# First MLP: on VectorE h times n of a tile follows the last Mish operation of the preceding tile; ScalarE copies x2 out behind the Exp of a group's last tile

## The chip, the cores and the metric

One core of a Trainium2 chip runs the whole program. The metric is the time of one execution on the device in microseconds (us), the median of the runs. TensorE (PE in the profile) multiplies, VectorE (DVE), ScalarE (ACT) and GpSimd (POOL) do the elementwise work, and SyncE (SP) issues most of the transfers.

## The reference, cut to what matters

```
x  = attention(q, k, v)            # 1536 tokens x 512, causal band of local keys and global keys
h  = x @ w_in                      # 512 -> 2048
g  = h * tanh(log1p(exp(h)))       # Mish
x2 = g @ w_out                     # 2048 -> 512
p  = domain_probs / sum(domain_probs)
for e in 4 experts:                # 512 -> 1024 -> 512
    out += p[:, e] * (relu(x2 @ w1[e]) @ w2[e])
```

The change lies in the first MLP alone, the three lines from h to x2.

## The kernel before

Each float32 matrix product is made from float16 high and low parts, as three products (high by high, high by low, low by high). After the attention, `rest` runs on every engine. The 1536 tokens form 3 groups (NG) of 512, and the 2048 columns of h form 16 tiles (FT) of 128; a tile of the first MLP is one of these 16 column tiles for one group, [128 x 512], so there are 48 (STEPS). All engines run the same loop, `for T in range(STEPS + LAG)` with LAG = 6, and each is in step T at a time of its own. Nothing is scheduled by a tool: every engine's order is the order of the code, and semaphores tie the engines together.

What is done for tile T, and in which step of which engine:

- PE, step T: the first product, 12 matmuls of 512 columns (L608), into PSUM bank T % 4. It waits until L1353 of tile T-4 has read that bank (b_ready).
- ACT, step T: L973, u = exp(h). DVE, step T: L1347, u = min(u, U_MAX); L1349, n = (u + 2) u; L1353, g = -h n, which reads h from PSUM and n from SBUF.
- ACT, step T+1: L989, r = ln(n + 2), and L991, r = exp(-r). DVE, step T+1: L1365 and L1367, one Newton step on r.
- POOL, in its own loop: L816, g = g r, as soon as L1367 of the tile is done. Its result is g of the tile.
- ACT, step T+2: L983, the float16 high part of g. DVE, step T+2: L1359, its low part.
- PE, step T+6: the second product, 12 matmuls (L677), which adds the tile's share of x2 into four PSUM banks of their own. It waits for L1359 (h_ready).

With the last tile of a group (tiles 15, 31, 47, at step 21, 37, 53) the four banks hold x2 of the group. `take_x2` has ACT copy them to SBUF (L946, four copies). The second product of the next group's first tile (tile 16 at step 22, tile 32 at step 38) waits for each bank's copy before it writes the bank (x2_taken).

Between these, DVE has extra work at the end of certain steps: in steps 6, 8, ... 20 one reduction over a piece of the first expert's weights (L1070), in step 8 also the four small operations of `shares`, in steps 22 to 25 and 38 to 41 the largest value of x2 (L1298), in step 25 and 29 some small scale computations, in steps 31 to 34 the low parts of x2 (L1290), in steps 33, 35, 40 and 42 low parts of expert weights (L1323). At steps 1 and 3 it makes low parts of x for groups 1 and 2 (L1216); the second product of tile 0 waits for the last of these.

After the loop the experts follow, nearly all of it matmuls (L608).

Of the kernel before, what the change touches and what calls it, by code (L numbers as in the profile page):

```python
# [17 lines left out]
ALU = mybir.AluOpType  # L18
# [18 lines left out]
def program(nc, q, k, v, n_global, n_local, w_in, w_out, probs, w1, w2, out):  # L37
# [7 lines left out]
    FT = FF // P  # L45
# [3 lines left out]
    NG = N // GN  # L49
# [23 lines left out]
    with ExitStack() as ctx:  # L73
# [30 lines left out]
        def psum(i, n=GN, at=0):  # L104

            c = 512 * (i % 2) + at
            return bank[i // 2][:, c:c + n]
# [87 lines left out]
        u_t, n_t, r_t, g_t = temps[0:2], temps[2:4], temps[4:6], temps[6:10]  # L195
# [76 lines left out]
        u_ready, n_step, n_ready, b_ready = sem("u_ready"), sem("n_step"), sem("n_ready"), sem("b_ready")  # L272
# [3 lines left out]
        g_ready, h_hi, h_ready = sem("g_ready"), sem("h_hi"), sem("h_ready")  # L276
# [16 lines left out]
        STEPS = NG * FT  # L293
        LAG = 6
# [10 lines left out]
        W0_LOW = [T + 1 for T in W0_HIGH[:PIECES // 2]] + W0_HIGH[PIECES // 2:]  # L305


        TAKE_X2 = [FT + LAG - 1]
        TAKE_X2_LATE = {2 * FT + LAG - 1: 1}
        X2_SCALE = 7  # L310
        X2_HIGH = 8

# [519 lines left out]
        def _(act):  # L832
# [98 lines left out]
            def rest(banded):  # L931
# [8 lines left out]
                def take_x2(g):  # L940

                    for c in range(DC):
                        act.wait_ge(x2_psum, DC * g + c + 1)
                        if g and c == 0:
                            act.wait_ge(x_ready, XN + DC * g)
                        act.copy(y32[:, c], psum(4 + c)).then_inc(x2_taken, 1)  # L946
# [17 lines left out]
                act.wait_ge(inv_ready, 1)  # L964

                for T in range(STEPS + LAG):
                    if T in TAKE_X2:
                        take_x2(TAKE_X2.index(T))
                    if T < STEPS:
                        act.wait_ge(h_psum, T + 1)  # L970
                        if T >= 2:
                            act.wait_ge(n_ready, T - 1)
                        act.activation(u_t[T % 2], psum(T % 4), ACT.Exp, scale=inv_h).then_inc(u_ready, 1)  # L973
                    else:
                        expert_high(0, 0, T - STEPS)
                    if T in TAKE_X2_LATE:
                        take_x2(TAKE_X2_LATE[T])
                    if 0 <= T - 2 < STEPS:
                        m = T - 2
                        act.wait_ge(g_ready, m + 1)  # L980
                        if m >= RING:
                            act.wait_ge(l2_done, m - RING + 1)
                        act.activation(hv[:, m % RING, 0, :], g_t[m % 4], ACT.Copy).then_inc(h_hi, 1)  # L983
                    if 0 <= T - 1 < STEPS:
                        m = T - 1
                        act.wait_ge(n_ready, m + 1)
                        if m >= 2:
                            act.wait_ge(g_ready, m - 1)
                        act.activation(r_t[m % 2], n_t[m % 2], ACT.Ln, bias=two).then_inc(l_ready, 1)  # L989
                        act.wait_ge(l_ready, m + 1)  # L990
                        act.activation(r_t[m % 2], r_t[m % 2], ACT.Exp, scale=-1.0).then_inc(r_ready, 1)  # L991
                    if T in TURN_AT:
                        for c in range(DC):
                            x_high(TURN_AT[T], c)
                    ready = x2_due(T, X2_HIGH)
                    if ready and ready[1] < DC:
                        x2_high(*ready)
                    if T in W0_HIGH:
                        expert_0_high(W0_HIGH.index(T))
# [18 lines left out]
        def _(dve):  # L1018
# [256 lines left out]
            def rest():  # L1275
# [67 lines left out]
                for T in range(STEPS + LAG):  # L1343
                    if T < STEPS:
                        u, n = u_t[T % 2], n_t[T % 2]
                        dve.wait_ge(u_ready, T + 1)
                        dve.tensor_scalar(u, u, U_MAX, None, ALU.min).then_inc(n_step, 1)  # L1347
                        dve.wait_ge(n_step, T + 1)
                        dve.scalar_tensor_tensor(n, u, 2.0, u, ALU.add, ALU.mult).then_inc(n_ready, 1)  # L1349
                        if T >= 4:  # L1350
                            dve.wait_ge(h_ready, T - 3)
                        dve.wait_ge(n_ready, T + 1)
                        dve.scalar_tensor_tensor(g_t[T % 4], psum(T % 4), -1.0, n, ALU.mult, ALU.mult).then_inc(b_ready, 1)  # L1353
                    else:
                        expert_low(0, 0, T - STEPS)
                    if 0 <= T - 2 < STEPS:
# [4 lines left out]
                    if 0 <= T - 1 < STEPS:  # L1361
                        m = T - 1
                        n, r = n_t[m % 2], r_t[m % 2]
                        dve.wait_ge(r_ready, m + 1)
                        dve.scalar_tensor_tensor(e_t, n, 2.0, r, ALU.add, ALU.mult).then_inc(e_ready, 1)  # L1365
                        dve.wait_ge(e_ready, m + 1)
                        dve.scalar_tensor_tensor(r, e_t, 2.0, r, ALU.subtract, ALU.mult).then_inc(q_ready, 1)  # L1367
                    if T in TURN_AT:
                        for c in range(DC):
                            x_low(TURN_AT[T], c)  # L1370
# [95 lines left out]
```

## Time and profile before

| | us |
|---|---|
| median of 3 runs (lowest to highest) | 910.69 (910.62 to 911.55) |
| the profiled execution, its own time | 911.57 |
| its span (first to last instruction) | 909.7 |
| PE busy | 874.2 (96%) |
| DVE busy | 501.0 (55%) |
| ACT busy | 316.3 (35%) |
| POOL busy | 263.6 (29%) |

The shares are averages over stages of different kinds: attention up to about 150 us, the first MLP from there to about 424 us, the experts to the end. Times in the rows below are microseconds from the start of the span. In a timeline a row is one instruction or several alike: start, duration, engine, line and operation, out<-in, count, and in brackets how long the engine stood idle before it and who released it. Durations on DVE and ACT overlap a little: the next instruction can start before the one in front has ended, so steps are best measured from start to start.

### The profile page before, as it was taken

To read this page: it belongs to the slowest core of one execution; us is meant where nothing else is said; L and a number is where in the kernel's file an instruction comes from. 1 tells how busy PE (TensorE), PEld (TensorE's weight loads), DVE (VectorE), ACT (ScalarE), POOL (GpSimd) and SP (SyncE) were. 2 spreads that over 40 slices of the span, in tenths; PEclk is the share of its full clock that TensorE was granted. 3 is DMA by queue.
4 is the path that set the end of the run, shared out by engine and by line. 5 is a ranking of instruction groups with operands and counts; after the bars stand their busy time and mean duration, and the time that the engine had idled before them with its cause. 6 is when DMAs were issued, how large, how long until landed. Compare 5 with 4: busy or idle time off the path is not lost.

```text
span 909.7 us, 12637 instructions
## 1 busy us (share of the span) xinstructions
PE 874.2 (96%) x4916; PEld 443.7 (49%) x4916; DVE 501.0 (55%) x1010; ACT 316.3 (35%) x597; POOL 263.6 (29%) x218
## 2 busy tenths in 40 slices
PE   6878999899999999999999999999999999999998
PEld 6666776444444444444444444444444444444443
DVE  7665887999999999984641224322134322212121
ACT  4798886544554555463020111101020101101020
POOL 1368993222222232220009400068000193000000
PEclk9898999999999999999999999999999999999999
DMA  9771320000000000202000400000400000000001
GB/s 222 244 251 39 124 99 1 1 1 1 1 7 3 1 1 1 93 3 93 4 6 0 180 6 1 6 0 8 177 1 2 4 0 0 1 24 23 35 12 49
DMA packets 52004, 39.19 MB, mean 43 GB/s; under 512 B 40816, under 2 KB 41712, under 8 KB 51440
## 3 DMA queue, kind: packets, MB, share of 16 engines
q1 hardware_dynamic: 49888, 34.31, 12.6%
q10 hardware_dynamic: 2064, 4.19, 1.3%
q8 instruction: 31, 0.51, 0.2%
q14 instruction: 21, 0.17, 0.1%
HBM read 35.35 MB, written 3.15 MB: 42 GB/s over the span
## 4 chain that ended last, share of the span: by engine, by line
PE 70%; DVE 20%; ACT 7%; issue 2%; POOL 0%; DVEq 0%; ACTq 0%
PE bank L608 58%; PE bank L677 5%; DVE tmp L1349 4%; DVE tmp L1367 3%; DVE xT L1365 3%; PE bank L547 2%; DVE tmp L1347 2%; PE bank L579 2%; ACT scaled L866 2%; DVE tmp L1353 2%; PE bank L598 2%; DVE hid L1359 1%; ACT tmp L989 1%; ACT tmp L850 1%; ACT tmp L891 1%
## 5 line engine op out<-in xcount | busy, mean ns | idle before, releaser
L962 ACT ACTIVATE hid<-bank 128x512 f16<-128x512 f32 x96 | 57.2, 596 | 413.8 <-PE bank L608 413.8
L608 PE MATMUL bank<-xT,wA 128*128 128x512 f16 (+1 forms) x864 | 194.6, 379 | 0.0
L1340 DVE SCALAR_TENSOR_TENSOR hid<-bank,hid 128x512 f16<-128x512 f32 x96 | 66.3, 691 | 177.2 <-ACT hid L962 177.2
L677 PE MATMUL bank<-hid,wB 128*128 128x512 f16 x576 | 133.8, 383 | 5.4 <-ACT acc L946 4.2
L608 PEld LDWEIGHTS bank<-xT,wA 128*128 128x128 f16 x864 | 84.5, 98 | 100.7 <-issue 0.2
L608 PE MATMUL bank<-wA,hid 128*128 128x512 f16 x576 | 125.3, 379 | 0.0
L608 PE MATMUL bank<-wB,hid 128*128 128x512 f16 x576 | 125.3, 379 | 0.0
L608 PE MATMUL bank<-xT,wB 128*128 x576 | 125.3, 379 | 0.0
L816 POOL TENSOR_TENSOR tmp<-tmp 128x512 f32<-128x512 f32 x48 | 67.8, 1412 | 195.8 <-DVE tmp L1367 195.8
L771 POOL TENSOR_SCALAR stage<-stage,sc 128x1024 f32<-128x1024 f32 x32 | 35.8, 1120 | 255.1 <-DVEq L1333 245.3
L1418 DVE SCALAR_TENSOR_TENSOR acc<-bank,pg,acc 128x512 f32<-128x512 f32 x36 | 27.0, 751 | 131.7 <-PE bank L608 131.7
L677 PEld LDWEIGHTS bank<-hid,wB 128*128 128x128 f16 x576 | 56.6, 99 | 75.2 <-DVE hid L1359 5.2
L608 PEld LDWEIGHTS bank<-wB,hid 128*128 128x128 f16 x576 | 56.4, 98 | 68.0
L608 PEld LDWEIGHTS bank<-xT,wB 128*128 128x128 f16 x576 | 56.4, 98 | 68.0
L608 PEld LDWEIGHTS bank<-wA,hid 128*128 128x128 f16 x576 | 56.3, 98 | 68.0
L983 ACT ACTIVATE hid<-tmp 128x512 f16<-128x512 f32 x48 | 30.3, 630 | 116.5 <-POOL tmp L816 116.5
L1231 DVE SCALAR_TENSOR_TENSOR tmp<-bank,tmp 128x384 f16<-128x384 f32 (+2 forms) x96 | 47.0, 490 | 34.2 <-ACT tmp L891 33.1
L608 PE MATMUL bank<-xT,hid 128*128 (+1 forms) x288 | 63.6, 379 | 0.0
L579 PE MATMUL bank<-ident,tmp 128*128 128x128 f32 x240 | 45.7, 290 | 8.7 <-DVE tmp L1231 6.6
L850 ACT ACTIVATE tmp<-tmp 128x288 f32<-128x288 f32 (+2 forms) x96 | 48.6, 507 | 15.5 <-DVE tmp L1120 14.4
L1349 DVE SCALAR_TENSOR_TENSOR tmp<-tmp 128x512 f32<-128x512 f32 x48 | 52.1, 1086 | 1.6
L608 PEld LDWEIGHTS bank<-xT,hid 128*128 128x128 f16 x288 | 28.2, 98 | 34.0
(111 smaller groups left out, 940.8 us busy)
## 6 DMA issues: line engine op xcount, KB each, us to landing
stage<-in_moe_w SPq DMA_DIRECT2D x8, 2048.0 KB, 9.9
stage<-in_moe_w_in SPq DMA_DIRECT2D x1, 4096.0 KB, 14.5
wB<-in_moe_w_out ACTq DMA_DIRECT2D x1, 4096.0 KB, 15.9
hid<-in_q SPq DMA_DIRECT2D x16, 192.0 KB, 3.3
hid<-in_k SPq DMA_DIRECT2D x16, 192.0 KB, 3.4
xT<-in_v SPq DMA_DIRECT2D x8, 384.0 KB, 4.9
out_y<-acc SPq DMA_DIRECT2D x12, 256.0 KB, 2.0
rows<-max SPq DMA_DIRECT2D x4, 128.0 KB, 3.8
```

The lines of the kernel that those rows point to most:

```text
L579: last = pe.transpose(dst[:, b * P:(b + 1) * P], src[:, b * P:(b + 1) * P], ident[:])
L608: last = pe.matmul(dst, lhs(c, a), rhs(c, b), start=(c == 0 and n == 0), stop=(c == chunks - 1 and n == 2))
L677: last = pe.matmul(psum(4 + d), w_out_s[:, a, f // 2, f % 2, d * P:(d + 1) * P], hv[:, T % RING, b, :], start=(f == 0 and n == 0), stop=(f ...
L771: pool.tensor_scalar(tmp, src, scale, 1.0, ALU.mult, ALU.mult).then_inc(w_part, 1)
L816: pool.tensor_tensor(g_t[T % 4], g_t[T % 4], r_t[T % 2], ALU.mult).then_inc(g_ready, 1)
L850: act.activation(t, t, ACT.Exp, bias=nmax[:, u:u + 1], scale=-1.0).then_inc(p_ready, 1)
L962: act.activation(hv[:, f, 0, :], psum(f % 4), ACT.Relu).then_inc(f_hi, 1)
L983: act.activation(hv[:, m % RING, 0, :], g_t[m % 4], ACT.Copy).then_inc(h_hi, 1)
L1231: dve.scalar_tensor_tensor(pt[:, 1], src, P_SCALE, pt[:, 0], ALU.mult, ALU.subtract).then_inc(pT_dve, 1)
L1340: dve.scalar_tensor_tensor(hv[:, f, 1, :], psum(f % 4), 0.0, hv[:, f, 0, :], ALU.max, ALU.subtract).then_inc(f_ready, 1)
L1349: dve.scalar_tensor_tensor(n, u, 2.0, u, ALU.add, ALU.mult).then_inc(n_ready, 1)
L1365: dve.scalar_tensor_tensor(e_t, n, 2.0, r, ALU.add, ALU.mult).then_inc(e_ready, 1)
```

## The change

On VectorE, L1353 (h times n of tile T) with its two waits moves inside step T from its place behind L1349 to a place behind L1359 and the two Newton operations L1365 and L1367 of tile T-1, and ahead of all of the step's extra work. On ScalarE, the four copies of x2 of group 0 move behind the Exp L973 of step 21; those of group 1 already stand behind the Exp of step 37, and stay there.

```diff
-        TAKE_X2 = [FT + LAG - 1]
-        TAKE_X2_LATE = {2 * FT + LAG - 1: 1}
+        TAKE_X2_AT = [(g + 1) * FT + LAG - 1 for g in range(NG - 1)]
...
                 for T in range(STEPS + LAG):
-                    if T in TAKE_X2:
-                        take_x2(TAKE_X2.index(T))
                     if T < STEPS:
                         act.wait_ge(h_psum, T + 1)
...
                         expert_high(0, 0, T - STEPS)
-                    if T in TAKE_X2_LATE:
-                        take_x2(TAKE_X2_LATE[T])
+                    if T in TAKE_X2_AT:
+                        take_x2(TAKE_X2_AT.index(T))
...
                         dve.scalar_tensor_tensor(n, u, 2.0, u, ALU.add, ALU.mult).then_inc(n_ready, 1)
-                        if T >= 4:
-                            dve.wait_ge(h_ready, T - 3)
-                        dve.wait_ge(n_ready, T + 1)
-                        dve.scalar_tensor_tensor(g_t[T % 4], psum(T % 4), -1.0, n, ALU.mult, ALU.mult).then_inc(b_ready, 1)
...
                         dve.scalar_tensor_tensor(r, e_t, 2.0, r, ALU.subtract, ALU.mult).then_inc(q_ready, 1)
+                    if T < STEPS:
+                        if T >= 4:
+                            dve.wait_ge(h_ready, T - 3)
+                        dve.wait_ge(n_ready, T + 1)
+                        dve.scalar_tensor_tensor(g_t[T % 4], psum(T % 4), -1.0, n_t[T % 2], ALU.mult, ALU.mult
+                                                 ).then_inc(b_ready, 1)
                     if T in TURN_AT:
```

The order on VectorE of two steps of the first MLP, one that ends with a weight reduction and the next, in the kernel before (L1353 is h times n):

```order
L1367 SCALAR_TENSOR_TENSOR tmp<-xT,tmp 128x512
L1070 TENSOR_REDUCE wpieces<-stage 128x1
L1347 TENSOR_SCALAR tmp<-tmp 128x512
L1349 SCALAR_TENSOR_TENSOR tmp<-tmp 128x512
L1353 SCALAR_TENSOR_TENSOR tmp<-bank,tmp 128x512
L1359 TENSOR_TENSOR hid<-tmp,hid 128x512
L1365 SCALAR_TENSOR_TENSOR xT<-tmp 128x512
L1367 SCALAR_TENSOR_TENSOR tmp<-xT,tmp 128x512
L1347 TENSOR_SCALAR tmp<-tmp 128x512
L1349 SCALAR_TENSOR_TENSOR tmp<-tmp 128x512
```

And the same place in the changed kernel, where the lines of before have new numbers: L1347 is L1344, L1349 is L1346, L1359 is L1352, L1365 is L1358, L1367 is L1360, L1070 is L1067, and h times n, L1353 before, is L1365 now:

```order
L1360 SCALAR_TENSOR_TENSOR tmp<-xT,tmp 128x512
L1365 SCALAR_TENSOR_TENSOR tmp<-bank,tmp 128x512
L1067 TENSOR_REDUCE wpieces<-stage 128x1
L1344 TENSOR_SCALAR tmp<-tmp 128x512
L1346 SCALAR_TENSOR_TENSOR tmp<-tmp 128x512
L1352 TENSOR_TENSOR hid<-tmp,hid 128x512
L1358 SCALAR_TENSOR_TENSOR xT<-tmp 128x512
L1360 SCALAR_TENSOR_TENSOR tmp<-xT,tmp 128x512
L1365 SCALAR_TENSOR_TENSOR tmp<-bank,tmp 128x512
L1344 TENSOR_SCALAR tmp<-tmp 128x512
```

The one operation that reads a PSUM bank has moved from between n and the low part of g to directly behind the last Newton operation, ahead of the reduction where there is one.

The order on ScalarE at step 21, where x2 of group 0 is copied out (L946), before:

```order
L991 ACTIVATE tmp<-tmp 128x512
L946 COPY acc<-bank 128x512 x4
L973 ACTIVATE tmp<-bank,sc 128x512
L983 ACTIVATE hid<-tmp 128x512
L989 ACTIVATE tmp<-tmp,sc 128x512
```

And now, with L988 for L991, L970 for L973, L945 for L946, L980 for L983 and L986 for L989:

```order
L988 ACTIVATE tmp<-tmp 128x512
L970 ACTIVATE tmp<-bank,sc 128x512
L945 COPY acc<-bank 128x512 x4
L980 ACTIVATE hid<-tmp 128x512
L986 ACTIVATE tmp<-tmp,sc 128x512
```

The Exp and the four copies have changed places; at step 37 the order is the latter in both kernels.

## Rows read from the trace of the kernel before

**Rows 1.** Windows: busy time (and instructions) of each engine, TensorE clock, DMA share, GB/s
```profile
339.00:347.00 8.00, 4.66 (x14) 1.83 (x15) 7.66 (x11) 6.83 (x12) 1.58 (x2) 0.79 0.00 0
424.00:909.00 485.00, 482.21 (x2235) 218.39 (x2232) 141.72 (x224) 57.20 (x96) 102.52 (x72) 1.00 0.08 25
```

**Rows 2.** Timeline of PE at the copies of group 0
```profile
252.29 2.75 PE L608 MATMUL bank<-xT,wA 128*128 128x512 f16 x12
255.93 2.75 PE L677 MATMUL bank<-hid,wB 128*128 128x512 f16 x12 [0.88 <-ACT acc L946]
258.51 2.75 PE L608 MATMUL bank<-xT,wA 128*128 128x512 f16 x12
```

**Rows 3.** Timeline of PE at the copies of group 1
```profile
336.21 2.75 PE L608 MATMUL bank<-xT,wA 128*128 128x512 f16 x12
...
342.34 4.44 PE L677 MATMUL bank<-hid,wB 128*128 128x512 f16 x12 [3.37 <-ACT acc L946]
...
346.61 2.75 PE L608 MATMUL bank<-xT,wA 128*128 128x512 f16 x12
```

**Rows 4.** Timeline of ACT at the copies of groups 0 and 1
```profile
255.22 2.03 ACT L946 COPY acc<-bank 128x512 f32<-128x512 f32 x4
257.11 0.72 ACT L973 ACTIVATE tmp<-bank,sc 128x512 f32<-128x512 f32 x1
...
341.62 2.04 ACT L946 COPY acc<-bank 128x512 f32<-128x512 f32 x4
```

**Rows 5.** Timeline of DVE and POOL, a step that ends with a reduction
```profile
246.14 0.69 DVE L1367 SCALAR_TENSOR_TENSOR tmp<-xT,tmp 128x512 f32<-128x512 f32 x1
246.75 1.21 DVE L1070 TENSOR_REDUCE wpieces<-stage 128x1 f32<-128x1024 f32 x1
...
246.91 1.27 POOL L816 TENSOR_TENSOR tmp<-tmp 128x512 f32<-128x512 f32 x1 [3.47 <-DVE tmp L1367]
...
247.88 0.58 DVE L1347 TENSOR_SCALAR tmp<-tmp 128x512 f32<-128x512 f32 x1
...
248.50 0.69 DVE L1349 SCALAR_TENSOR_TENSOR tmp<-tmp 128x512 f32<-128x512 f32 x1
...
250.50 0.68 DVE L1365 SCALAR_TENSOR_TENSOR xT<-tmp 128x512 f32<-128x512 f32 x1
```

**Rows 6.** Timeline of DVE, POOL and ACT, the plain step behind it
```profile
251.22 0.69 DVE L1367 SCALAR_TENSOR_TENSOR tmp<-xT,tmp 128x512 f32<-128x512 f32 x1
251.83 0.42 DVE L1347 TENSOR_SCALAR tmp<-tmp 128x512 f32<-128x512 f32 x1
251.99 1.38 POOL L816 TENSOR_TENSOR tmp<-tmp 128x512 f32<-128x512 f32 x1 [3.81 <-DVE tmp L1367]
...
252.28 1.64 DVE L1349 SCALAR_TENSOR_TENSOR tmp<-tmp 128x512 f32<-128x512 f32 x1
...
253.40 0.63 ACT L983 ACTIVATE hid<-tmp 128x512 f16<-128x512 f32 x1 [2.71 <-POOL tmp L816]
...
254.03 0.69 DVE L1353 SCALAR_TENSOR_TENSOR tmp<-bank,tmp 128x512 f32<-128x512 f32 x1
254.63 0.68 DVE L1359 TENSOR_TENSOR hid<-tmp,hid 128x512 f16<-128x512 f32 x1
254.68 0.63 ACT L991 ACTIVATE tmp<-tmp 128x512 f32<-128x512 f32 x1
...
255.34 0.69 DVE L1365 SCALAR_TENSOR_TENSOR xT<-tmp 128x512 f32<-128x512 f32 x1
```

**Rows 7.** Timeline of DVE and POOL at step 1, low parts of x
```profile
158.51 2.48 DVE L1216 TENSOR_TENSOR xT<-bank,xT 128x512 f16<-128x512 f32 x4
158.67 1.27 POOL L816 TENSOR_TENSOR tmp<-tmp 128x512 f32<-128x512 f32 x1 [15.34 <-DVE tmp L1367]
```

**Rows 8.** Waits from 145 to 450 us
```profile
PE bank L677 <- DVE xT L1216: 1.2, 1, 1.2
```

**Rows 9.** Timeline of DVE at step 31, behind a low part of x2 (L1290)
```profile
314.25 1.49 DVE L1347 TENSOR_SCALAR tmp<-tmp 128x512 f32<-128x512 f32 x1
```

## The prediction, made before the changed kernel was run

> **What bounds the kernel now.** I read the windows first. From 424 us to the end PE is busy for 482.21 of 485.00 us at full clock [rows 1], and nothing that the change touches lies there: that part moves as a block with the end of the first MLP. So only idle PE time before 424 us can be won. The timeline of PE shows how much there is. From one first product to the next, with a second product between, PE takes (336.21 - 258.51) / 15 = 5.18 us per step [rows 2, 3], and that is its own pace, with no gap inside. Two steps are longer. Around the second product of tile 16: 258.51 - 252.29 = 6.22 us, so **1.04 us** is lost, behind a wait for the x2 copies L946 [rows 2]. Around that of tile 32: 346.61 - 336.21 = 10.40 us, so **5.22 us** is lost [rows 3]. Of this, 3.37 us is again the wait for L946; then the 12 matmuls take 4.27 us instead of 2.59, since the granted clock, 1.00 elsewhere, has a mean of 0.79 in this window [rows 1]: after the idle time it is at the lower of its two levels (1.2 against 2.4 GHz) for a while. Both waits are for ACT, and ACT is late because DVE, POOL and ACT together run behind PE. How late is seen in the copies: the first group's start at 255.22 us and the second's at 341.62 [rows 4], while PE wants the first bank at 252.29 + 2.59 = 254.88 and at 336.21 + 2.59 = 338.80 us. The start of the MLP holds 1.2 us more, a wait of the first second product for L1216 [rows 8]. So the pace of the DVE-POOL-ACT group up to step 37 decides, and PE's own pace after that.
>
> **What paces DVE, POOL and ACT.** A step that ends with a reduction takes 251.22 - 246.14 = 5.08 us from L1367 to L1367 [rows 5, 6]. The plain one behind it takes 255.34 - 251.22 = 4.12 us up to L1365, and L1367 follows L1365 by 0.72 us [rows 5, 6], so 4.84 us.
>
> In the plain step a ring through three engines closes: L1367 starts, POOL 0.77 us later, for 1.38 us; L983 starts 0.03 us after POOL has ended, L991 another 1.28 us later, L1365 another 0.66, L1367 another 0.72: 4.84 us [rows 6]. DVE is not free meanwhile: L1349 takes 1.64 us instead of 0.69, and ends 0.55 us after POOL [rows 5, 6]. DVE is held while POOL runs. L1347 is held in the same way when POOL has begun first: in the reduction step L1349 starts 0.32 us after the end of POOL, although L1347 was next from 247.88 us on [rows 5]. The reduction is not held, and neither is L1216, which reads one operand from PSUM: four take 2.48 us, 0.62 each, with POOL at work in 1.27 us of it [rows 7].
>
> **The change on VectorE, step by step.** No instruction is added or removed. L1353 reads PSUM and one SBUF tile, as L1216 does, so I take it as not held by POOL. It now stands directly behind L1367, the time in which POOL runs. Set L1367's start to 0:
>
> - Plain step: L1353 starts at 0.61. POOL runs from 0.77 to 2.04, with 1.27 us, because no L1347 is in front of it. L1347 is held; L1349 starts at 2.04 + 0.32 = 2.36, L1359 0.61 later at 2.97, and L1365 could start at 3.57. The ring allows it at 0.77 + 1.27 + 0.03 + 1.28 + 0.66 = 4.01. The step is 4.01 + 0.72 = **4.73 us**, 0.11 less than 4.84. DVE gets idle time of 0.4 us in it.
> - Reduction step: L1353 at 0.61, reduction at 1.22, L1347 at 1.22 + 1.13 = 2.35 (not held, POOL is over), L1349 at 2.80, L1359 at 3.41, L1365 at 4.01. Also **4.73 us**, 0.35 less than 5.08.
>
> Another small saving is inside: before, L1353 waited for L1349 in front of it and started 0.11 us after its end (253.92 to 254.03), so 0.69 + 0.11 = 0.80 us from start to start, where an instruction that depends on nothing in front follows in 0.60 (254.03 to 254.63) [rows 6]. With L1359 behind L1349, 0.61 us is taken, some 0.18 us less in steps that DVE alone paces. The Trainium skill (VectorE: DVE Perf Modes, section The DRAIN you can't avoid) speaks against this: it says that a semaphore between VectorE operations costs nothing extra, as the pipe has to empty anyway. By that rule the 0.18 us would not exist, and the reduction step would come to 4.91 us; the rows here show it, and I go by them. The result is the same by either.
>
> The Trainium skill (SBUF — State Buffer, section SBUF: two separate sides) says that VectorE and GpSimd share a port pair as an exclusive lock, which a VectorE operation needs when it has two SBUF inputs or is in a two-port mode. By that rule, L1353 with one SBUF input is free of the lock. The trace agrees for L1216 [rows 7]; for L1353 itself no row of before shows it, since it never ran beside POOL.
>
> **Does the first stall go?** From step 4 to step 20 there are 7 steps with a reduction and 9 plain ones ahead of the copies (step 8 counted as an ordinary one): 7 x 0.35 + 9 x 0.11 = 3.4 us earlier. On ACT the Exp L973 is now in front of the copies, 0.57 us at most (four copies in 2.03, so the Exp's slot is of that size [rows 4]). Copies start at 255.22 - 3.4 + 0.6 = 252.4, the first is over at 253.0, and PE wants it at 254.88. The stall is gone with 1.9 us to spare, so 1.04 us is won. The Exp's own input is there, since the first product of tile 21 ended one second product before 252.29, at 249.7.
>
> **Does the second?** PE will be 1.3 us earlier there (1.04 and the 0.3 below), and wants the first bank at 337.5, so the copies must start by 336.9: 4.7 us sooner than 341.62. Available: 3.4 us, another 0.35 for step 20, and 15 steps to step 36 at no less than 0.11: 5.4 us. Most of these save more: behind low parts of x2, L1347 took 1.49 us [rows 9], held behind a POOL that itself had been made to wait. With such steps like the reductions, at 0.35 or more, the sum is 8 to 10 us. More than about 8 can't be used, as L973 then waits for PE. So the stall goes, and with it the low clock: 5.22 us.
>
> **The start.** L1216 of step 3 comes two steps into the loop. Its gain lies between nothing and two reduction-like savings, 0.7 us, and L1353 of step 3 now stands ahead of it; I take 0.3.
>
> **What could be late next.** L1353 frees the PSUM bank for the first product four tiles on. It comes about 2.4 us later in its step, but the steps come earlier; L1353 of the tile at 254.03 is wanted by PE about three steps, 15 us, later. Nothing queued behind it waits for anything new: its two waits are for DVE's own earlier work. The copies no longer hold up the Exp of step 21. SP and POOL queues are not touched. From step 38 on DVE must keep 5.18 us per step on average; with 4.73 and some longer steps it does.
>
> **Sum.** 0.3 + 1.04 + 5.22 = 6.6 us off the profiled execution: 911.57 - 6.6 = 905.0, span 903.1. The median of the runs was 0.88 us below the profiled one; if that difference stays, 904.1. It may have been a shorter time at the low clock, which goes away now. I forecast **904.6**.
>
> **Rivals.**
>
> 1. *L1353 is held by POOL too (slower).* Place: each step. It would end 0.55 us after POOL, at 2.59. A plain step is then about 4.9 us, a reduction step 2.55 + 1.13 + 0.45 + 0.61 + 0.60 + 0.72 = 6.06, 1.0 us longer than now. Seven of them and nine at +0.1 make 7.9 us by step 21; the stall before tile 16 grows from 0.9 to 9.4 us, and about 2 more are lost up to step 37: some 921. It decides against the change once L1353 takes more than about 1.3 us. For it: L1349 and L1347 are held. Against: L1216. Chance 0.06.
> 2. *Only part of the second stall goes.* If later steps save the 0.11 alone and the reductions only half of what I think, copies start about 3 us earlier, and 1 to 2 us of stall is left, with or without the low clock: 906 to 909. Chance 0.09.
> 3. *Nothing is won.* The ring at 4.84 also paces the steps in which DVE gets faster, and the Exp in front of the first copies costs 0.6 us: 910.7 to 911.3. Against: reduction steps at 5.08 are longer than the ring. Chance 0.04.
>
> The forecast has 0.81.
>
> **Numbers.** This kernel's measurement can tell about 0.2% (1.8 us) from no change. Faster by more: 0.81 + 0.09 = 0.90, less a little for the upper end of rival 2: 0.89. Within it 0.05, slower 0.06. The likeliest case's own range is 903.6 to 905.6: from a start gain of 0.7 on the lowest run, 910.62 - 7.0, to no start gain on the profiled execution, 911.57 - 6.3, and a bit. For 8 in 10 and a bit of rival 2, I give 903.5 to 907.0.
>
> **What would show it right or wrong.** Right: h times n at 0.69 us right behind the last Newton operation, beside POOL; POOL at 1.27; L1347 held instead of L1349; plain and reduction steps both near 4.73; DVE with small waits for ACT's second Exp; no PE wait for the copies at either group, clock 1.00 there; PE's second products 5.18 us apart all through. Wrong: h times n at 1.4 us; a PE wait for b_ready, or for the copies at the second group; or a stall in the experts that was hidden before, for instance a weight split that ends late.

## The result, and the profile after

| | before | changed |
|---|---|---|
| median, us (lowest to highest) | 911.12 (910.62 to 911.56, 4 runs) | 903.62 (902.35 to 904.85, 4 runs) |
| the profiled execution, its own time | 911.57 | 902.35 |
| its span | 909.7 | 900.5 |
| DVE busy | 501.0 | 483.3 |
| POOL busy | 263.6 | 257.6 |

The ratio on record is 0.9922, with a 95% interval of 0.991 to 0.9935 (the two medians divided give 0.9918): 0.8% faster. 904.6 was forecast, within 903.5 to 907.0. The median of the kernel before is now over four runs; it was 910.69 over three when the forecast was made.

The timeline of PE at the copies of group 0, in the changed kernel (L607 is the first product, L676 the second, L945 the copy):

```profile
249.56 2.75 PE L607 MATMUL bank<-xT,wA 128*128 128x512 f16 x12
252.15 2.75 PE L676 MATMUL bank<-hid,wB 128*128 128x512 f16 x12
254.74 2.75 PE L607 MATMUL bank<-xT,wA 128*128 128x512 f16 x12
```

The second product of tile 16 follows the first product of tile 22 at once: 5.18 us from first product to first product, where it was 6.22 [rows 2]. Around the copies of group 1 it is the same:

```profile
332.44 2.75 PE L607 MATMUL bank<-xT,wA 128*128 128x512 f16 x12
...
335.03 1.24 PE L676 MATMUL bank<-hid,wB 128*128 128x512 f16 x5
```

(the window ends inside the second product, so that five of its matmuls are counted). There is no wait, where [rows 3] have 3.37 us, and no time at the lower clock, where [rows 1] have a mean of 0.79. Two windows of the changed kernel over this place (length, then busy time and count of PE, PE's weight loads, DVE, ACT and POOL, then the granted clock):

```profile
330.00:340.00 10.00, 10.00 (x49) 4.50 (x47) 7.38 (x12) 7.32 (x12) 2.54 (x2) 1.00 0.00 0
340.00:350.00 10.00, 10.00 (x48) 4.58 (x47) 9.11 (x16) 6.16 (x9) 2.54 (x2) 1.00 0.01 2
```

Why ACT is in time is seen in a reduction step and the plain one behind it. Timeline of DVE, POOL and ACT in the changed kernel (L1360 is the last Newton operation, L1365 h times n, L1067 the reduction, L1344 the minimum, L1346 n, L1352 the low part of g, L1358 the first Newton operation):

```profile
229.74 0.69 DVE L1360 SCALAR_TENSOR_TENSOR tmp<-xT,tmp 128x512 f32<-128x512 f32 x1
230.35 0.68 DVE L1365 SCALAR_TENSOR_TENSOR tmp<-bank,tmp 128x512 f32<-128x512 f32 x1
230.51 1.27 POOL L815 TENSOR_TENSOR tmp<-tmp 128x512 f32<-128x512 f32 x1 [3.46 <-DVE tmp L1360]
230.95 1.21 DVE L1067 TENSOR_REDUCE wpieces<-stage 128x1 f32<-128x1024 f32 x1
...
232.08 0.42 DVE L1344 TENSOR_SCALAR tmp<-tmp 128x512 f32<-128x512 f32 x1
...
234.48 0.69 DVE L1360 SCALAR_TENSOR_TENSOR tmp<-xT,tmp 128x512 f32<-128x512 f32 x1
235.09 0.68 DVE L1365 SCALAR_TENSOR_TENSOR tmp<-bank,tmp 128x512 f32<-128x512 f32 x1
235.25 1.27 POOL L815 TENSOR_TENSOR tmp<-tmp 128x512 f32<-128x512 f32 x1 [3.47 <-DVE tmp L1360]
235.69 1.11 DVE L1344 TENSOR_SCALAR tmp<-tmp 128x512 f32<-128x512 f32 x1
236.55 0.63 ACT L980 ACTIVATE hid<-tmp 128x512 f16<-128x512 f32 x1 [2.26 <-POOL tmp L815]
236.83 0.69 DVE L1346 SCALAR_TENSOR_TENSOR tmp<-tmp 128x512 f32<-128x512 f32 x1
...
238.49 0.69 DVE L1358 SCALAR_TENSOR_TENSOR xT<-tmp 128x512 f32<-128x512 f32 x1 [0.37 <-ACT tmp L988]
239.22 0.69 DVE L1360 SCALAR_TENSOR_TENSOR tmp<-xT,tmp 128x512 f32<-128x512 f32 x1
```

h times n takes 0.68 us with POOL beside it; the n that took 1.64 us [rows 6] takes 0.69. In the plain step POOL now holds the minimum, 1.11 us, and DVE has 0.37 us left over before ACT's second Exp is ready. From L1360 to L1360 both steps take 4.74 us, where they took 5.08 and 4.84 [rows 5, 6].

**Where the time went, in three pieces.** A profile can be cut at three rows: the start of the attention's last scores product (PE L547, now L546), the start of the first second product, and the start of the first second product of expert 0. PE's timeline of the kernel before has:

```profile
143.31 0.84 PE L547 MATMUL bank<-hid 64*128 64x256 f32 x8 [0.45 <-DVE tmp L1120]
...
172.00 2.76 PE L677 MATMUL bank<-hid,wB 128*128 128x512 f16 x12 [1.15 <-DVE xT L1216]
...
429.49 2.75 PE L608 MATMUL bank<-wA,hid 128*128 128x512 f16 x12
```

And in the changed kernel:

```profile
140.94 0.84 PE L546 MATMUL bank<-hid 64*128 64x256 f32 x8 [0.45 <-DVE tmp L1117]
...
169.26 2.76 PE L676 MATMUL bank<-hid,wB 128*128 128x512 f16 x12 [0.92 <-DVE xT L1213]
...
420.50 11.82 PE L607 MATMUL bank<-wA,hid 128*128 128x512 f16 x54
```

The start of the MLP went from 28.69 to 28.32 us (0.37 less), its main part from 257.49 to 251.24 (6.25 less). The span is 9.2 us shorter; 2.4 of that lie ahead of the first of the cuts, in the attention, and 0.2 behind the last. Neither of these two belongs to the change, as the repeats below show.

### The profile page after: what moved, and what is told of

Read it like the earlier page. It is cut to its first block, busy times and chain, and to the rows that moved or that the text cites. A ratio compares the mean times of both kernels' runs of the same rounds, so it can differ in the third digit from the quotient of the medians.

```text
span 900.5 us, 12637 instructions
## 1 busy us (share of the span) xinstructions
PE 873.6 (97%) x4916; PEld 444.9 (49%) x4916; DVE 483.3 (54%) x1010; ACT 319.2 (35%) x597; POOL 257.6 (29%) x218
## 4 chain that ended last, share of the span: by engine, by line
PE 89%; ACT 5%; DVE 4%; issue 1%; POOL 0%; DVEq 0%
PE bank L607 67%; PE bank L676 14%; PE bank L546 2%; PE bank L578 2%; ACT scaled L865 2%; PE bank L597 2%; ACT tmp L849 1%; ACT tmp L890 1%; PE bank L501 1%; DVE xT L1213 1%; PE bank L559 1%; DVE tmp L1117 1%; ACT hid L839 0%; DVE tmp L1228 0%; DVE tmp L1346 0%
## 5 line engine op out<-in xcount | busy, mean ns | idle before, releaser
L607 PE MATMUL bank<-xT,wA 128*128 128x512 f16 (+1 forms) x864 | 194.6, 379 | 0.0
L607 PEld LDWEIGHTS bank<-xT,wA 128*128 128x128 f16 x864 | 84.5, 98 | 100.6
L676 PE MATMUL bank<-hid,wB 128*128 128x512 f16 x576 | 132.2, 379 | 0.9 <-DVE xT L1213 0.9
L607 PE MATMUL bank<-xT,wB 128*128 x576 | 125.3, 379 | 0.0
L607 PE MATMUL bank<-wA,hid 128*128 128x512 f16 x576 | 125.3, 379 | 0.0
L607 PE MATMUL bank<-wB,hid 128*128 128x512 f16 x576 | 125.3, 379 | 0.0
L815 POOL TENSOR_TENSOR tmp<-tmp 128x512 f32<-128x512 f32 x48 | 61.4, 1280 | 190.2 <-DVE tmp L1360 190.2
L676 PEld LDWEIGHTS bank<-hid,wB 128*128 128x128 f16 x576 | 56.3, 98 | 69.1 <-DVE xT L1213 1.4
L607 PEld LDWEIGHTS bank<-xT,wB 128*128 128x128 f16 x576 | 56.4, 98 | 67.9
L607 PEld LDWEIGHTS bank<-wA,hid 128*128 128x128 f16 x576 | 56.4, 98 | 68.0
L607 PEld LDWEIGHTS bank<-wB,hid 128*128 128x128 f16 x576 | 56.3, 98 | 68.0
L607 PE MATMUL bank<-xT,hid 128*128 (+1 forms) x288 | 63.6, 379 | 0.0
L980 ACT ACTIVATE hid<-tmp 128x512 f16<-128x512 f32 x48 | 30.2, 629 | 67.6 <-POOL tmp L815 67.5
L607 PEld LDWEIGHTS bank<-xT,hid 128*128 128x128 f16 x288 | 28.2, 98 | 34.0
L970 ACT ACTIVATE tmp<-bank,sc 128x512 f32<-128x512 f32 x48 | 32.6, 682 | 33.9 <-PE bank L607 30.8
```

Source lines behind the costliest of these rows:

```text
L607: last = pe.matmul(dst, lhs(c, a), rhs(c, b), start=(c == 0 and n == 0), stop=(c == chunks - 1 and n == 2))
L676: last = pe.matmul(psum(4 + d), w_out_s[:, a, f // 2, f % 2, d * P:(d + 1) * P], hv[:, T % RING, b, :], start=(f == 0 and n == 0), stop=(f ...
L815: pool.tensor_tensor(g_t[T % 4], g_t[T % 4], r_t[T % 2], ALU.mult).then_inc(g_ready, 1)
```

## The experiments

Each was timed on a chip together with the kernel before, and the ratio is to the runs of the kernel before on that same chip, not to the first row. "Start" and "main" are the two pieces above from its profile, "attention" the time of the first cut.

| run | median us (n) | ratio to before [95%] | attention | start | main |
|---|---|---|---|---|---|
| before | 911.12 (4) | 1 | 143.31 | 28.69 | 257.49 |
| before_again | 910.41 (12) | 1.0 [0.9991, 1.001] | 141.30 | 28.69 | 257.53 |
| changed | 903.62 (4) | 0.9922 [0.991, 0.9935] | 140.94 | 28.32 | 251.24 |
| again | 904.08 (6) | 0.9929 [0.9917, 0.9941] | 141.32 | 28.33 | 251.24 |
| again2 | 904.68 (5) | 0.994 [0.9927, 0.9954] | 143.14 | 28.33 | 251.24 |
| dve_only | 904.33 (5) | 0.9932 [0.9919, 0.9945] | 140.90 | 28.34 | 251.24 |
| act_only | 910.14 (12) | 0.9997 [0.9987, 1.0007] | 140.98 | 28.70 | 257.39 |
| behind_low | 905.89 (6) | 0.9943 [0.9931, 0.9955] | 143.14 | 28.57 | 252.34 |
| slack8 | 904.55 (5) | 0.9933 [0.9919, 0.9946] | 142.86 | 28.32 | 251.24 |
| slack14 | 906.38 (4) | 0.9959 [0.9944, 0.9974] | 141.31 | 28.32 | 253.73 |
| slack16 | 912.98 (7) | 1.0027 [1.0016, 1.0038] | 141.02 | 28.32 | 260.51 |
| low_first | 903.19 (5) | 0.992 [0.9905, 0.9935] | 140.98 | 27.72 | 251.24 |
| low_before_newton | 906.33 (5) | 0.995 [0.9936, 0.9964] | 143.73 | 28.28 | 252.92 |
| step3_early | 902.64 (5) | 0.9912 [0.9899, 0.9926] | 143.05 | 26.88 | 251.28 |

### What varies without a change: again, again2, before_again

The same two kernels once more, with no edit. What was expected of the changed kernel:

> The changed kernel once more, to see what varies without a change. In its profile the span from the start of the second product of tile 0 to the end was 731.2 us against 737.7 before (6.5 us less); the 2.4 us beyond that which its span was shorter came from before 40 us, inside the attention, where before's trace shows 6.8 us at the lower TensorE clock (32.3 to 39.2 us of its clock record) and the changed kernel's does not. Theory 1: that part varies from run to run, the 6.5 do not. Then this profile has 731.2 again within 0.1, its attention differs by up to 3 us, and the timed runs lie between 902 and 905.5. Rival: the attention has become shorter for good; then all runs lie near 902.5.

and, later, beside step3_early:

> The changed kernel a third time, on the same chip as step3_early, to compare the two. From the last attention product to PE's last instruction 756.3 us within 0.05, as in both profiles so far; timed runs within 902 to 905.5.

Of the kernel before:

> The kernel before once more. Theory 1: from the start of the second product of tile 0 to the end 737.7 us within 0.1 if the time at the lower clock behind the second wait is the same, up to 1.7 us less if it is not; its attention up to that point may be up to 3 us longer or shorter than the 172.0 of the first profile. Both copies' waits are there.

Measured: main 251.24 in all three profiles of the changed kernel, and 257.49 and 257.53 in the two of before, with both waits for the copies each time. The attention ended at 140.94, 141.32 and 143.14 us in one kernel and at 143.31 and 141.30 in the other. So the 2.4 us do not come from the change: one and the same kernel shows 2 us between its profiles there, and the change's own part is the 6.6 us of start and main. The 0.2 us behind the last cut are of the same kind: that piece takes 480.2 us in one profile of the kernel before and 480.0 in the other. Theory 1 of the first expectation holds. One run of again2, at 905.55 us, lies just above the range expected for it.

What differs in the attention is seen in the granted clock. The window from 30 to 40 us, in before and then in before_again (the clock is the third number from the end):

```profile
30.00:40.00 10.00, 8.35 (x84) 6.53 (x80) 5.99 (x26) 5.68 (x15) 1.54 (x2) 0.66 1.01 395
```

```profile
30.00:40.00 10.00, 9.36 (x106) 7.69 (x107) 8.36 (x33) 8.17 (x19) 0.00 (x0) 0.83 0.99 382
```

The 14 profiles of the table fall in two groups by this window. Where its clock is 0.83 or 1.00, the attention ends between 140.90 and 141.32 us; where it is 0.66 or 0.51, between 142.86 and 143.73. The changed kernel's first profile isn't free of the lower clock, as the expectation has it: it has 1.00 here, and 0.66 from 50 to 60 us. What decides where the clock falls is open. A median of few runs depends on how many of them fall in each group: the four of the changed kernel are 902.35, 902.79, 904.45 and 904.85, and their median lies in the gap.

### One half of the change at a time: dve_only, act_only

dve_only puts the four copies of group 0 ahead of the Exp again (cut to what matters, as are the diffs below):

```diff
+                    if T in TAKE_X2:
+                        take_x2(TAKE_X2.index(T))
                     if T < STEPS:
                         act.wait_ge(h_psum, T + 1)
...
```

> Only the move on VectorE; the copies of group 0 stand ahead of the Exp again. Theory 1: VectorE's steps carry all of it; the copies start some 0.6 us earlier than in the changed kernel, where PE already had 3 us to spare. Same time as the changed kernel within 0.3 us, both waits of PE for the copies absent. The Exp of step 21 starts 1.4 us later. Rival: the order on ScalarE is needed to remove the first wait; then 1 us slower than the changed kernel.

act_only puts h times n back, and has only the move on ScalarE:

```diff
                         dve.scalar_tensor_tensor(n, u, 2.0, u, ALU.add, ALU.mult).then_inc(n_ready, 1)
+                        if T >= 4:
+                            dve.wait_ge(h_ready, T - 3)
+                        dve.wait_ge(n_ready, T + 1)
+                        dve.scalar_tensor_tensor(g_t[T % 4], psum(T % 4), -1.0, n, ALU.mult, ALU.mult).then_inc(b_ready, 1)
...
```

> Only the move on ScalarE; h times n stands in its old place. Theory 1: the copies of group 0 come 0.57 us later and PE's first wait grows from 0.9 to 1.4 or 1.5 us; the second wait, 5.2 us with its low clock, shrinks by as much or stays. Time of before or up to 0.5 us more. Rival: the Exp that starts earlier lets VectorE start earlier and gives a gain of 0.5 us or more.

Measured: dve_only has start and main of the changed kernel to 0.02 us. The move on VectorE is the whole gain; the one on ScalarE adds nothing to it. (The Exp of step 21 starts 2.4 us later there, at 250.22 instead of 247.85, and not 1.4 as expected; it costs nothing.) act_only shows what the latter does by itself. PE's timeline at both copies:

```profile
254.20 2.75 PE L676 MATMUL bank<-hid,wB 128*128 128x512 f16 x12 [1.47 <-ACT acc L945]
...
340.06 4.30 PE L676 MATMUL bank<-hid,wB 128*128 128x512 f16 x12 [2.81 <-ACT acc L945]
```

The first wait is 0.59 us longer than in [rows 2], since the Exp now runs first; the second is 0.56 shorter than in [rows 3], since PE comes to it that much later while ACT comes no later: its copies start 169.66 us behind the first second product, and 169.62 before. Main differs by 0.1 us, the time by nothing that can be measured.

### Which part of the saving is POOL, which the dependent pair: behind_low

h times n stands between the low part of g and the Newton operations:

```diff
                         dve.tensor_tensor(hv[:, m % RING, 1, :], g_t[m % 4], hv[:, m % RING, 0, :], ALU.subtract
                                           ).then_inc(h_ready, 1)
+                    if T < STEPS:
+                        ...
+                        dve.scalar_tensor_tensor(g_t[T % 4], psum(T % 4), -1.0, n_t[T % 2], ALU.mult, ALU.mult
+                                                 ).then_inc(b_ready, 1)
                     if 0 <= T - 1 < STEPS:
...
```

> The changed kernel, but h times n stands between the low part of g and the Newton operations, so not beside GpSimd's product, and no longer directly behind the n on which it depends. It takes apart the two savings. Theory 1: the savings come from filling the time in which GpSimd holds VectorE. Here the next minimum goes ahead of GpSimd and n is held for 1.64 us as before. Plain steps stay at 4.84 us, reduction steps are 4.90 (0.18 less than 5.08, from the pair that no longer waits). Gain per step 0 and 0.18 instead of 0.11 and 0.35: by step 21 about 1.3 us, the first wait goes down to 0.2 or less, the second from 3.4 to some 0 to 1.5 us. Time 905 to 908. Rival: the dependent pair alone makes the gain; then it equals the changed kernel.

Its timeline (L1366 is the last Newton operation here, L1358 h times n):

```profile
229.91 0.69 DVE L1366 SCALAR_TENSOR_TENSOR tmp<-xT,tmp 128x512 f32<-128x512 f32 x1
230.52 0.42 DVE L1344 TENSOR_SCALAR tmp<-tmp 128x512 f32<-128x512 f32 x1
230.68 1.38 POOL L815 TENSOR_TENSOR tmp<-tmp 128x512 f32<-128x512 f32 x1 [3.62 <-DVE tmp L1366]
230.97 1.64 DVE L1346 SCALAR_TENSOR_TENSOR tmp<-tmp 128x512 f32<-128x512 f32 x1
...
232.76 0.69 DVE L1352 TENSOR_TENSOR hid<-tmp,hid 128x512 f16<-128x512 f32 x1
```

n is held for 1.64 us again. Plain steps take 4.85 us, reduction steps 4.88: h times n, which no longer waits for the instruction directly in front of it, saves 0.20 of the 0.34 us in a reduction step and nothing in a plain one, and the place beside POOL saves the rest. This is one way to divide the saving; no run has the place beside POOL without the other part. PE's wait at group 0 is down to 0.08 us (a second product starts at 254.67, 2.67 us after the first product at 252.00, where 2.59 is PE's own pace), and that at group 1 is there still:

```profile
338.58 2.75 PE L676 MATMUL bank<-hid,wB 128*128 128x512 f16 x12 [0.87 <-ACT acc L945]
```

Behind it the clock stays up (1.00 from 336 to 346 us). Start and main are 1.35 us longer than in the changed kernel, and 5.3 shorter than before. The savings per step are small, but the smaller part of them already removes 5.3 of the 6.6 us, since it shortens the second wait enough for the clock to stay up; the last 1.35 us need the place beside POOL too.

### How much VectorE has to spare: slack8, slack14, slack16

More reductions of [128 x 1024], with results that nothing uses, at the end of steps 22 to 29 (slack8: one each), 22 to 35 (slack14: one each), 22 to 29 (slack16: two each):

```diff
+                    if T in range(22, 30):
+                        for _ in range(1):
+                            dve.tensor_reduce(sc[:, 60:61], stage[:, 0:PIECE], AX_X, ALU.max)
```

> The changed kernel with one more reduction (1.13 us on VectorE, its result unused) at the end of each of steps 22 to 29: eight. Theory 1: PE is the bound and VectorE has some 4 to 5 us to spare by step 37. The reductions make steps 22 to 24 longer by 0.6 us each, 25 and 29 by 1.13, and 26 to 28 by nothing, since they fit beside the ring: 4.1 us in all, no wait of PE for the copies or one under 0.5 us; time that of the changed kernel. Rival: VectorE is still the bound; then 4 us or more slower.

> The changed kernel with the additional reduction in each of steps 22 to 35: fourteen. Theory 1: 4.1 us as with eight, and 1.13 in each of steps 31 to 35: 9.8 us, some 5 more than there is to spare. PE waits about 5 us for the copies of group 1, and runs at the lower clock behind it (1.7 us): time 6 to 7 us more than the changed kernel. Rival: hidden; same time.

> The changed kernel with two additional reductions in each of steps 22 to 29. Theory 1: steps 22 to 24 longer by 1.73 each, 25 and 29 by 2.26, 26 to 28 by 1.13: 13.1 us, PE waits some 8 us and then has 1.7 at the lower clock: about 10 us slower than the changed kernel. Rival: PE waits at b_ready or for low parts of g instead of for the copies.

Measured, as the time from the first second product to L1360 of tile 35: 3.9 us more than in the changed kernel with slack8, 8.95 with slack14, 12.9 with slack16 (4.1, 9.8 and 13.1 were worked out; with slack14 the last of its reductions lengthens its step by 0.49 us and not by 1.13). slack8 costs PE nothing, 251.24. The copies of group 1 start at 334.17 us there, 2.8 us ahead of the second product that needs the first of them:

```profile
334.17 2.04 ACT L945 COPY acc<-bank 128x512 f32<-128x512 f32 x4
```

slack14 and slack16 make PE wait for the copies:

```profile
337.90 2.75 PE L676 MATMUL bank<-hid,wB 128*128 128x512 f16 x12 [2.33 <-ACT acc L945]
```

```profile
342.03 5.10 PE L676 MATMUL bank<-hid,wB 128*128 128x512 f16 x12 [5.82 <-ACT acc L945]
```

slack14 costs 2.49 us, of which 2.33 are this wait. slack16 costs 9.27: 5.82 us of wait for the copies, 0.76 for h times n of a tile (b_ready, the rival's place, in a small part), 2.35 because the 12 matmuls behind the wait take 4.94 us instead of 2.59 (clock 0.68 from 341 to 350 us, and not the 1.7 us that were taken for it), and 0.3 in small pieces. So some 6 us are to spare, not the 4 to 5 expected: 3.9 + 2.8 less 0.6 for the first copy with slack8, 8.95 - 2.33 = 6.6 with slack14. slack14 came out 4 us faster than forecast for this, and because the clock did not fall. In the changed kernel only part of it can be seen directly: the copies of group 1 start 4.3 us ahead of the second product that needs the first of them, behind an Exp that itself waited for PE:

```profile
330.05 0.69 ACT L970 ACTIVATE tmp<-bank,sc 128x512 f32<-128x512 f32 x1 [2.18 <-PE bank L607]
330.70 2.53 ACT L945 COPY acc<-bank 128x512 f32<-128x512 f32 x4
```

That PE is the bound between the two copies is shown by the dose that costs nothing.

### The start of the MLP: low_first, low_before_newton, step3_early

What is left of PE's idle time in the MLP are the waits for the low parts of x: 1.26 us ahead of PE's transposes for the next group of x (L509), and 0.92 ahead of the first second product; the change put h times n ahead of these low parts. low_first puts it behind them:

```diff
+                    if T in TURN_AT:
+                        for c in range(DC):
+                            x_low(TURN_AT[T], c)
                     if T < STEPS:
                         ...
                         dve.scalar_tensor_tensor(g_t[T % 4], psum(T % 4), -1.0, n_t[T % 2], ALU.mult, ALU.mult
                                                  ).then_inc(b_ready, 1)
-                    if T in TURN_AT:
-                        for c in range(DC):
-                            x_low(TURN_AT[T], c)
```

> The changed kernel, but in steps 1 and 3 the four low parts of x come ahead of h times n. Both steps' low parts start 0.61 us earlier, and PE waits for both (1.3 us ahead of the transposes, 0.9 us ahead of the second product of tile 0). Theory 1: the second product of tile 0 starts 0.6 us earlier and all behind it too, since VectorE has time to spare at both copies: 0.6 us faster than the changed kernel. Rival: the later h times n holds up the first product of a tile; no gain.

low_before_newton puts them ahead of L1358 and L1360 too, in steps 1 and 3:

```diff
+                    if T in TURN_AT:
+                        for c in range(DC):
+                            x_low(TURN_AT[T], c)
                     if 0 <= T - 1 < STEPS:
                         m = T - 1
...
-                    if T in TURN_AT:
-                        for c in range(DC):
-                            x_low(TURN_AT[T], c)
```

> The changed kernel, but in steps 1 and 3 the low parts of x come ahead of the Newton operations too. They start 1.4 to 1.9 us earlier than in the changed kernel, at once when ScalarE's high parts are there, so both waits of PE at the start go: up to 2.2 us (1.3 and 0.9). GpSimd, ScalarE and VectorE's ring start 2.4 us later in each of the two steps. Theory 1: VectorE had 3 us to spare at the copies of group 0; with PE 2 us earlier and the ring up to 3 us later, PE waits there for 1 to 2 us, and the sum is a gain of 0.5 to 1.5 us against the changed kernel. Rival: no wait there, gain of 2 us.

Measured: low_first gains 0.60 us in the start and loses nothing in main. The wait ahead of the transposes is 0.67 us instead of 1.26, the one ahead of the first second product is 0.92 as before, since PE comes earlier too. low_before_newton failed: start and main are 1.64 us longer than in the changed kernel, and its median is 906.33 where slack8, on the same chip, has 904.55. ACT, DVE and PE in its step 3:

```profile
168.85 2.04 ACT L927 ACTIVATE xT<-bank 128x512 f16<-128x512 f32 x4
169.47 2.48 DVE L1213 TENSOR_TENSOR xT<-bank,xT 128x512 f16<-128x512 f32 x4 [0.84 <-ACT xT L927]
...
172.01 4.45 PE L676 MATMUL bank<-hid,wB 128*128 128x512 f16 x12 [2.34 <-DVE xT L1213]
```

The wait ahead of the transposes is gone, but step 1 held up the ring. ACT reaches the high parts of group 2 (L927) only at 168.85, which is 25.12 us behind the first cut, where the changed kernel has 23.73, and the low parts have to wait for them. So they start where they did (25.74 us behind the cut, 25.79 in the changed kernel), while PE comes 1.3 us earlier: the two waits have become one. I had worked out when DVE could start and not when ACT would have the input. PE waits 2.34 us and then is at the lower clock, so that 12 matmuls take 4.27 us; main is 1.68 longer for this. There was no wait at the copies of group 0, where I expected the loss. (The 4 us in the next expectation compare times in two profiles whose attention differs by 2.8 us; the high parts are 1.4 us later.)

So only step 3 should be changed in this way, step3_early:

```diff
+                    if T == 3:
+                        for c in range(DC):
+                            x_low(TURN_AT[T], c)
                     if 0 <= T - 1 < STEPS:
...
+                    if T == 1:
+                        for c in range(DC):
+                            x_low(TURN_AT[T], c)
                     if T < STEPS:
...
-                    if T in TURN_AT:
-                        for c in range(DC):
-                            x_low(TURN_AT[T], c)
```

> As low_first in step 1, but in step 3 the four low parts of x stand ahead of the Newton operations of tile 2. low_before_newton got slower because its step 1 held the ring back, so that ScalarE's high parts of group 2 came 4 us later; here step 1 is as in low_first and these high parts come at the same time as there. Theory 1: the low parts start 0.8 us earlier (when the first high part is there), PE's wait of 0.9 us ahead of the second product of tile 0 goes to about 0.1, and all behind it moves 0.8 us: from the last attention product to PE's last instruction 0.8 us less than low_first and 1.4 less than the changed kernel. The ring is about 1.7 us later from step 3 on, and VectorE has over 5 us to spare. Rival: the ring's delay opens the wait at the copies of group 0; no gain.

Measured: start 26.88, which is 0.84 less than low_first and 1.45 less than again2, main 251.28. The wait ahead of the first second product is gone:

```profile
166.78 2.04 ACT L927 ACTIVATE xT<-bank 128x512 f16<-128x512 f32 x4
167.39 2.48 DVE L1213 TENSOR_TENSOR xT<-bank,xT 128x512 f16<-128x512 f32 x4 [0.85 <-ACT xT L927]
...
169.93 2.76 PE L676 MATMUL bank<-hid,wB 128*128 128x512 f16 x12
```

Its median is 2.0 us below that of the changed kernel on the same chip (902.64 against 904.68), of which start and main explain 1.4; the rest is within what the attention varies by from run to run. The ring is 1.6 us later from step 3 on, as expected, which the spare time hides. It is the fastest version measured, at 0.9912 [0.9899, 0.9926] of before. The intervals of changed, again and low_first overlap with it, and only that of again2, on its chip, does not; so what puts it ahead is above all the 1.4 us in the profile.

## Why the prediction was right, point by point

- **The bound.** The PE time lost at the two copies was 1.04 and 5.22 us, 6.26 in all; main got shorter by 6.25. What lies behind the last cut moved as a block: it takes 480.2 us before (909.7 - 429.49) and 480.0 in the changed kernel (900.5 - 420.50). Right. "1.00 elsewhere" for the clock holds from 150 us on; in the attention it was down to 0.66 in the window shown above, which the forecast did not look at.
- **The steps.** 4.73 us was worked out for both kinds, 4.74 measured. h times n is not held by POOL, POOL takes 1.27 us, the minimum is held instead of n. Right. The pair that waited for its neighbour was taken as worth 0.18, measured 0.20 with behind_low. The Trainium skill (VectorE: DVE Perf Modes, section The DRAIN you can't avoid) says of a row of copies that a semaphore between VectorE operations costs nothing extra. Here it does where the wait is for the instruction directly in front: 0.80 us from start to start instead of 0.60 [rows 6]. In behind_low the same wait still stands in the code, one instruction later, and that 0.20 us is gone. The runs do not tell the cost of the semaphore from that of the result's way to the next instruction.
- **First wait.** Gone with DVE's half of the change alone. The copies started at 248.42 us in the changed kernel, so the first was over at 248.9, and PE wanted it at 252.15: 3.2 us to spare for an estimate of 1.9. Counted from the first cut, the copies came 4.4 us earlier, and 2.8 were worked out (3.4 less 0.6 for the Exp). The term for the steps ahead was too small: up to the last Newton operation of tile 19 the ring gained 5.0 us and not 3.4. It left out what steps 1 to 3 save, 1.16 us, and took step 8, which has `shares` beside its reduction, at 0.35, where it saved 0.79.
- **Second wait and clock.** Gone. Counted from the first cut, the copies came 8.6 us earlier, and the ring had gained 10.6 us by the last Newton operation of tile 35, for an estimate of 8 to 10 of which about 8 could be used. The spare time at this place is about 6 us. The steps with low parts of x2 saved more than the 0.35 that was their lower bound, 0.63 us each. The L1347 that took 1.49 us there [rows 9] stands in an order in which the low part goes first and POOL takes longer:

```profile
313.59 0.74 DVE L1290 SCALAR_TENSOR_TENSOR xT<-acc,sc,xT 128x512 f16<-128x512 f32 x1
313.75 1.71 POOL L816 TENSOR_TENSOR tmp<-tmp 128x512 f32<-128x512 f32 x1 [3.46 <-DVE tmp L1367]
```

In the changed kernel POOL goes first and takes 1.27 us, the low part takes 1.38 us and the next minimum 0.41, and such a step takes 4.89 instead of 5.52 us:

```profile
308.80 1.27 POOL L815 TENSOR_TENSOR tmp<-tmp 128x512 f32<-128x512 f32 x1 [3.62 <-DVE tmp L1360]
309.24 1.38 DVE L1287 SCALAR_TENSOR_TENSOR xT<-acc,sc,xT 128x512 f16<-128x512 f32 x1
310.54 0.41 DVE L1344 TENSOR_SCALAR tmp<-tmp 128x512 f32<-128x512 f32 x1
```

- **The start.** 0.3 us was taken, 0.37 measured. That L1353 would now stand ahead of the low parts was named; that this costs 0.6 us, more than the gain, was not: low_first shows it. So 0.3 came out nearly right with a cost of 0.6 us left out, and without that cost the start would have gained 0.97.
- **From the profile to the median.** The part that was wrong. I put the 0.88 us between the profiled execution and the median down, as a possibility, to less time at the lower clock behind the second wait, and took off 0.4 us for it. In before_again that time is all there and main is the same, and the attention is 2.0 us shorter; it is the attention that varies. With the fourth run the difference was no longer 0.88 but 0.45 us. The changed kernel's profiled execution was forecast at 905.0 us and took 902.35; of the 2.65 us between them, 2.4 are the attention. The time fell in the range partly by luck: the range has no term for the attention, the median of 903.62 is 0.12 us inside its lower end, and two of the four runs, 902.35 and 902.79, lie below it. What the prediction had right is the 6.6 us of start and main, measured as 6.62.
- **The rivals.** That POOL holds h times n is refuted by its 0.68 us. Part of the second wait remains in behind_low, which has the pair's saving alone, and not in the changed kernel. The move on ScalarE costs nothing and brings nothing, with and without the other.

## What to carry to other kernels

Where two engines hold each other, look at which instruction stands where the hold happens. Here a VectorE operation with one input in PSUM and one in SBUF could fill the time of a GpSimd product (0.68 us beside it). Moving it there saved 0.11 us in a plain step, 0.34 in one with a reduction and 0.63 in one with a low part of x2, with no instruction less. An engine that is a little late all along shows itself only at the few places where the bound engine waits for it, so the gain is the sum of those waits and the clock lost behind them, not that of the steps; what the steps save beyond it is spare time, and a dose of useless work tells how much. When an operation is moved ahead, ask when its input comes, and who else in the ring is held up for it.

## What the runs showed of the hardware

After an idle time of PE the clock fell in some cases and not in others of the same length: not after 2.33 us (slack14, clock 1.00 in its window, 12 matmuls in 2.58 us), but after 2.34 us (low_before_newton, a mean of 0.79 in its window), and each time after 2.81 us and more (act_only 2.81, before 3.37, before_again 3.40, slack16 5.82). The two windows, of slack14 and of low_before_newton:

```profile
330.00:350.00 20.00, 17.67 (x83) 7.86 (x82) 19.01 (x29) 10.51 (x19) 4.92 (x4) 1.00 0.00 0
```

```profile
170.00:178.00 8.00, 5.99 (x20) 2.37 (x21) 7.54 (x13) 3.92 (x7) 1.26 (x1) 0.79 0.00 0
```

So a wait near this length can cost 1.7 us more or nothing, and the idle time alone does not tell which. Otherwise one and the same code repeated its main part within 0.04 us from profile to profile, while the attention ahead of it moved by over 2 us between profiles of one kernel, with a granted clock of 0.66 from 30 to 40 us in the longer ones and 0.83 or 1.00 in the shorter ones.
